# Attention, routed experts and a gated layer on one core: tokens stay in expert order for the gated stage, y turned by VectorE

## What is computed

```
kv  = einsum('bhsd,bhse->bhde', k, v)           # per batch and head, 64x64
o   = q @ kv;  x = o / sqrt(mean(o*o) + 1e-6) * g_norm       # N x 512
logits = x @ w_gate + modality_bias[modality_id]             # 8 experts
e = argmax(logits);  gate_w = softmax(logits)[e]
y[t] = gate_w[t] * (relu(x[t] @ w1[e]) @ w2[e])              # w1 512x1024
out = (sigmoid(y @ wg_gate) * (y @ wg_val)) @ w_out          # 512x1536, 1536x512
```

## Time and profile before

| | |
|---|---|
| three runs | 1637.22 to 1642.83 us, median 1638.06 |
| the profiled execution: span, first to last instruction | 1628.0 us; the runs' time also holds what lies before and after it, 10.1 us by the median |
| TensorE busy (its weight loads) | 1547.1 us, 95% (1297.4 us, 80%), 7924 instructions |
| VectorE, ScalarE, GpSimd busy | 559.8 us (34%), 397.9 us (24%), 181.3 us (11%) |
| first and second gated product (lines 1047, 1058) in the chain that ended last | 36% and 18% |

### The profile page before, as it was taken

How to read it: one execution, slowest core, us unless ns; L and a number is a source line. 1 busy time by engine, 2 the same in 40 slices (tenths; PEclk the granted TensorE clock), 3 DMA queues, 4 the chain that set the end, 5 groups by cost and what they waited for, 6 DMA issues and landing times.

```text
span 1628.0 us, 23019 instructions
## 1 busy us (share of the span) xinstructions
PE 1547.1 (95%) x7924; PEld 1297.4 (80%) x7925; DVE 559.8 (34%) x938; ACT 397.9 (24%) x744; POOL 181.3 (11%) x298
## 2 busy tenths in 40 slices
PE   6988479999999999969999999999999999999998
PEld 5878368888888888858888888888888888888886
DVE  2877743364524552233312212122121221212111
ACT  2766112222222222233221211112111121111111
POOL 1443122222222222100000000000000000000000
PEclk9999589999999999989999999999999999999999
DMA  9998223243314332043110000101001010010000
GB/s 226 257 266 232 81 75 106 71 154 129 120 47 136 112 128 64 31 134 103 65 52 1 30 23 1 53 1 52 1 1 52 1 52 1 0 52 0 27 0 26
DMA packets 56321, 120.61 MB, mean 74 GB/s; under 512 B 7614, under 2 KB 32190, under 8 KB 55488
## 3 DMA queue, kind: packets, MB, share of 16 engines
q1 hardware_dynamic: 49856, 99.75, 20.9%
q0 software_dynamic: 6400, 19.93, 4.0%
HBM read 91.33 MB, written 29.38 MB: 74 GB/s over the span
## 4 chain that ended last, share of the span: by engine, by line
PE 58%; issue 25%; DMA 6%; POOL 4%; POOLq 3%; DVE 1%; SPq 1%; ACT 0%; DVEq 0%; ACTq 0%
PE ps L1047 36%; PE ps L1058 18%; DMA vt<-in_v 4%; POOL xg L477 3%; POOLq L476 2%; PE ps L942 1%; PE ps L911 1%; PE ps L1037 1%; DMA raw<-in_moe_w 1%; POOL hold L471 1%; POOL from_now L475 1%; POOLq L484 0%; DMA x_rows<-xb 0%; DVE ssum L714 0%; POOL y_rows L485 0%
## 5 line engine op out<-in xcount | busy, mean ns | idle before, releaser
L1047 PE MATMUL ps<-yhi,gv 128*128 128x512 f32 x1728 | 548.1, 389 | 1.5 <-DVE ylo L874 1.5
L1047 PEld LDWEIGHTS ps<-yhi,gv 128*128 128x128 f32 x1728 | 324.3, 188 | 69.2 <-issue 1.9
L1047 PE MATMUL ps<-ylo,gv 128*128 128x512 f32 x864 | 336.1, 389 | 0.0
L1058 PE MATMUL ps<-wo,shi 128*128 128x512 f32 x864 | 266.9, 390 | 1.4 <-DVE slo L892 1.4
L890 DVE TENSOR_TENSOR s<-ps,sig 128x512 f32<-128x512 f32 x108 | 74.7, 692 | 489.2 <-ACT sig L609 489.2
L992 PE MATMUL ps<-ew,xhi 128*128 x640 | 203.3, 399 | 2.2 <-DVE xlo L811 1.7
L1014 PE MATMUL ps<-ew,hhi 128*128 x640 | 197.2, 389 | 1.3 <-DVE hlo L822 1.3
L1058 PEld LDWEIGHTS ps<-wo,shi 128*128 128x128 f32 x864 | 161.5, 188 | 35.0 <-DVE slo L892 1.9
L1047 PEld LDWEIGHTS ps<-ylo,gv 128*128 128x128 f32 x864 | 162.2, 188 | 33.7
L609 ACT ACTIVATE sig<-ps 128x512 f32<-128x512 f32 x108 | 64.7, 599 | 500.5 <-PE ps L1047 500.5
L1058 PE MATMUL ps<-wo,slo 128*128 128x512 f32 x432 | 168.2, 389 | 0.0
(11 more groups left out here) (139 smaller groups left out, 1280.0 us busy)
## 6 DMA issues: line engine op xcount, KB each, us to landing
raw<-in_moe_w SPq DMA_DIRECT2D x64, 512.0 KB, 4.0
qt<-in_q SPq DMA_DIRECT2D x8, 1152.0 KB, 13.3
x_rows<-xb SPq DMA_DIRECT2D x8, 1152.0 KB, 15.0
yin<-y_rows SPq DMA_DIRECT2D x18, 512.0 KB, 5.5
out<-ot SPq DMA_DIRECT2D x18, 512.0 KB, 2.9
kt<-in_k SPq DMA_DIRECT2D x7, 1152.0 KB, 20.2
vt<-in_v SPq DMA_DIRECT2D x7, 1152.0 KB, 25.1
graw<-in_moe_w_gate SPq DMA_DIRECT2D x6, 512.0 KB, 3.6
```

What stands on the lines that cost most here:

```text
L1047: last = mm(ps[:, 2 * (f % 2) + part, :], gv[f // 2][:, w, part, d, cols], x[c % 2][:, d, :], start=first, stop=end)
L1058: last = mm(ps[:, 4 + m, :], s[:, rows], wo[f // 2][:, w, f % 2], start=(f == 0 and s is shi and w == 0), stop=(f == GC - 1 and s is slo))
```

## The change

- The 4608 rows of `y_rows` now lie in **expert order with the padding closed up**: row = place in the padded list minus the padding of the experts before. `compact_rows` works out `to_i` (five VectorE operations after xlo of tile 0). The scatter stores beside each row of y its token number in `row_tok`, by a second indirect DMA.
- **The gate** is applied to the expert tile, when y is copied out of PSUM. For that GpSimd gathers the 128 gates of a tile (`gather_gate`), and the gather of x two tiles on waits for it, since it overwrites `from_now`. The copy also writes the row in the order (g, c, i), 4 groups of 4x32 features.
- **y is turned by VectorE** in squares of 32x32 (`y_turned`): a block is loaded with 32 tokens by 4 groups on the partitions (four DMAs, runs of 512 B), and four transposes give `yt` in SBUF. TensorE's transposes and their special order go.
- **Block 0** is loaded, turned and split within the expert stage, after step 35 (`ahead_of`; ScalarE issues the loads). The first weight piece is loaded once all tiles but the last expert's are done, the second right after the first is split. `high` and `low` of a piece stand after the column instead of before it.
- **Output rows** are scattered to their tokens by four indirect DMAs per block, with `out_tok` loaded from `row_tok` (128x36 elements of 4 bytes).

```diff
@@ SP
-            sp.dma_start(gate_n[:], gates.rearrange("(b p m) -> p b m", p=128, m=4)).then_inc(gates_in, 16)
...
             def load_y(b):
-                for half in range(2):
-                    wait(sp, pe_yt, 4 * (b - 1) + 2 * half + 2)
-                    sp.dma_start(yin[:, half], y_v[bass.ds(b, 1), :, 2 * half:2 * half + 2, :].rearrange("a p m d -> p (a m) d")).then_inc(yin_in[half], 16)
+                sp.wait_ge(yt_made, 4 * b)
+                for g in range(4):
+                    sp.dma_start(yin[32 * g:32 * g + 32], y_v[b, g]).then_inc(yin_in, 16)
...
-            sp.wait_ge(pe_hT, tiles_used * 2)
+            tiles_early = sp.value_load(used[0:1, 1:2], min_val=E - 1, max_val=NT)
+            sp.wait_ge(pe_y, tiles_early)
             load_glu(0)
+            load_glu(1)
             sp.wait_ge(pe_y, tiles_used)
             for p in range(2):
-                sp.wait_ge(y_out[p], (tiles_used + (1 - p)) // 2 * 16)
-            load_y(0)
-            for n in range(1, PIECES):
+                sp.wait_ge(y_out[p], (tiles_used + (1 - p)) // 2 * 32)
+            load_glu(2)
+            sp.dma_start(out_tok[:], row_tok_v, allow_slow_non_contiguous=True).then_inc(tok_in, 16)
+            load_y(1)
+            for n in range(3, PIECES):
                 load_glu(n)
...
@@ GpSimd
             def gather(t):
+                wait(pool, gate_in[t.p], 16 * t.half)
                 when(pe_x, t.n - 1)
...
             def scatter(t):
                 when(y_made, t.n + 1)
                 nc.gpsimd.tensor_copy(to_now[:, t.p:t.p + 1], to_i[:, bass.ds(t.n, 1)])
+                nc.gpsimd.tensor_copy(tok_now[:, t.p:t.p + 1], from_i[:, bass.ds(t.n, 1)])
                 pool.drain()
                 nc.gpsimd.indirect_dma_start(
                     out=y_rows, out_offset=bass.IndirectOffsetOnAxis(ap=to_now[:, t.p:t.p + 1], axis=0),
                     in_=y[:, t.p], in_offset=None, bounds_check=N - 1, oob_is_err=False).then_inc(y_out[t.p], 16)
+                nc.gpsimd.indirect_dma_start(
+                    out=row_tok, out_offset=bass.IndirectOffsetOnAxis(ap=to_now[:, t.p:t.p + 1], axis=0),
+                    in_=tok_now[:, t.p:t.p + 1], in_offset=None, bounds_check=N - 1, oob_is_err=False).then_inc(y_out[t.p], 16)
+
+            def gather_gate(t):
+                nc.gpsimd.indirect_dma_start(
+                    out=gate_now[:, t.p:t.p + 1], out_offset=None, in_=gates,
+                    in_offset=bass.IndirectOffsetOnAxis(ap=from_now[:, t.p:t.p + 1], axis=0)).then_inc(gate_in[t.p], 16)
...
                     use(Tile(i, c - 1), scatter)
+                    use(Tile(i, c + 1), gather_gate)
...
+            pool.wait_ge(tok_in, 16)
+            for b in range(NB):
+                for m in range(4):
+                    pool.wait_ge(o_kept, 4 * b + m + 1)
+                    nc.gpsimd.indirect_dma_start(
+                        out=out, out_offset=bass.IndirectOffsetOnAxis(ap=out_tok[:, 4 * b + m:4 * b + m + 1], axis=0),
+                        in_=ot[:, m], in_offset=None).then_inc(o_out[m], 16)
@@ ScalarE
+            def load_first():
+                for p in range(2):
+                    act.wait_ge(y_out[p], 32 * ((BLK // 128 + E) // 2))
+                for g in range(4):
+                    act.dma_start(yin[32 * g:32 * g + 32], y_v[0, g]).then_inc(yin_in, 16)
+                y_high(0, 0)
@@ VectorE
             def y_of(t):
-                wait(dve, y_out[t.p], 16 * t.half)
+                wait(dve, y_out[t.p], 32 * t.half)
                 dve.wait_ge(pe_y, t.n + 1)
-                nc.vector.tensor_copy(y[:, t.p], ps[:, 5, :]).then_inc(y_made, 1)
+                dve.wait_ge(gate_in[t.p], 16 * (t.half + 1))
+                nc.vector.tensor_scalar(y[:, t.p].rearrange("p (g c i) -> p c g i", g=4, c=DC),
+                                        ps[:, 5, :].rearrange("p (c g i) -> p c g i", g=4, c=DC),
+                                        gate_now[:, t.p:t.p + 1], None, ALU.mult).then_inc(y_made, 1)
...
+            def y_turned(i, c):
+                b = 2 * i + c
+                dve.wait_ge(yin_in, 64 * (b + 1))
+                for m in range(4):
+                    nc.vector.transpose(yt[c % 2][:, :, 128 * m:128 * m + 128].rearrange("p c (t j) -> p t c j", j=32),
+                                        yin[:, 4 * m:4 * m + 4, :].rearrange("p t (c i) -> p t c i", i=32)).then_inc(yt_made, 1)
...
-                    if f == 8 and not last:
-                        y_gated(i, c + 1)
+                    if f == 9 and not last:
+                        dve.wait_ge(glo_made, 3 * PIECES)
+                        y_turned(i, c + 1)
```

More of the change, by code:

```diff
@@ L210, in moe_program @@
     assert glu.at <= ew_base + UNITS * 2 * 4096
-    yhi0 = glu("yhi0", [128, DC, BLK], F32R)
-    ylo0 = glu("ylo0", [128, DC, BLK], F32R)
-    yhi, ylo = [yhi0, yhi1], [ylo0, ylo1]
+    ahead = Place(SBUF_END - 3 * DC * BLK * 4)
+    assert ahead.at >= expert_place.at
+    yt1 = Place(glu.at - DC * BLK * 4)("yt1", [128, DC, BLK], F32)
+    yt0 = Place(ahead.at)("yt0", [128, DC, BLK], F32)
+    ylo0 = ahead("ylo0", [128, DC, BLK], F32R)
+    yhi0 = ahead("yhi0", [128, DC, BLK], F32R)
+    yin = ahead("yin", [128, BLK // 32, 128], F32)
+    yhi, ylo, yt = [yhi0, yhi1], [ylo0, ylo1], [yt0, yt1]
     low_part = Place(glu_base)
@@ L227, in moe_program @@
     slo = small("slo", [128, BLK], F32R)
-    yin = small("yin", [128, 2, 2, D])
-    ot = small("ot", [128, 2, 2, D])
+    ot = small("ot", [128, 4, D])
+    assert glu.at <= SBUF_END - 3 * DC * BLK * 4
     ctx = ExitStack()
@@ L332, in __call__, with tiles @@
                         stage(t, *args)
-        def tiles(engine, step):
+        def tiles(engine, step, ahead_of=None):
             step(0, 0, False)
@@ L339, in tiles @@
                     step(i, c, True)
-            for n in range(FULL - 1, NT + 1):
+            step(0, FULL - 1, True)
+            if ahead_of:
+                ahead_of()
+            for n in range(FULL, NT + 1):
                 step(0, n, True)
@@ L601, in block_step @@
                 for f in range(GC):
-                    if first and f % 2 == 0 and f // 2 + 1 < PIECES:
-                        high(f // 2 + 1)
                     if f == 10 and not last:
@@ L612, in block_step @@
                     nc.scalar.copy(shi[:], s32[:]).then_inc(shi_made, 1)
+                    if first and f % 2 == 0 and f // 2 + 1 < PIECES:
+                        high(f // 2 + 1)
                     if f == 0 and not first:
@@ L781, in _ @@
                 one_hot(r_low, r_lo, 128, n, 1).then_inc(hot_made, 1)
+            then(nc.vector.scalar_tensor_tensor(out=r_spare[:], in0=r_nt[:], scalar=128.0, in1=ps[:, 1, 0:E], op0=ALU.mult, op1=ALU.subtract))
             dve.wait_ge(pe_table, 1)
@@ L892, in block_step @@
                     nc.vector.tensor_tensor(slo[:], s32[:], shi[:].bitcast(F32), ALU.subtract).then_inc(slo_made, 1)
+                    if first and f % 2 == 0 and f // 2 + 1 < PIECES:
+                        low(f // 2 + 1)
             low(0)
-            dve.wait_ge(gates_in, 16)
-            y_gated(0, 0)
-            y_low(0, 0)
             blocks(dve, block_step)
@@ L1029, in _ @@
             tiles(pe, tile_step)
-            def y_transposed(i, c, half):
-                b = 2 * i + c
-                pe.wait_ge(yg_made, 4 * b + 2 * half + 2)
-                for m in range(2 * half, 2 * half + 2):
-                    for d in range(DC):
-                        last = nc.tensor.transpose(ps[:, m, 128 * d:128 * d + 128], yin[:, half, m % 2, 128 * d:128 * d + 128], ident[:])
-                    last.then_inc(pe_yt, 1)
             def gate_value(i, c, f):
```

144 lines of the change are left out of this document (69 added, 75 removed).

## The result

The changed kernel takes **1836.19 us** (median of 4 runs, 1829.23 to 1837.71), the kernel before 1637.64 us (4 runs, 1635.13 to 1642.83: the three of the first section and one beside the changed kernel): a ratio of **1.121**, 95% interval 1.118 to 1.125. That is 12% slower, where 1622.7 was predicted, and outside the range.

The account below looks back on a forecast made before the run. TensorE was taken as the bound, busy for 487.2 of 489 us in the expert stage. Terms -14.3 - 12.0 + 1 + 3.5 + 5 + 1.4 from 1628.0 gave 1612.6, carried over to 1622.7 us; range 1610 to 1648.

Parts of the forecast that it names:

- Scatter, two small indirect DMAs, gather: Expert stage, GpSimd: the added small DMAs issue x later, delaying some tiles with weight loads; +5 us, bounds 0 and 22.
- d: Expert stage: excess of x's arrival over 12.07 us after the hold, delaying every second step by d; forecast 0.33 us.
- The text's own signs of being wrong: Row_tok 3 us behind y, expert steps over 13 us, TensorE waiting in block 0, or expert stage growing over 25 us.
- The clock: Seam to the gated stage: a clock drop during the new standstill slows some matmuls; +1 us, bounds 0 and 3.
- Transposes: Gated stage: TensorE's 16 transposes of y go in 8 block changes, VectorE's replacements cost nothing; -14.3 us.
- The seam: Between expert and gated stages: block 0 and weights ready early, shortening TensorE's standstill; -12.0 us, bounds -10 and -12.5.
- Block 0 loaded early: Tile 36 of the expert stage: work queues behind block 0's loads and transposes, delaying ReLU; +3.5 us, bounds 0 and 6.
- Tail: End of the kernel: four indirect stores replace two plain ones; +1.4 us, bounds 0.5 and 8.
- Carried over: Whole kernel: the 10.1 us by which the median of three runs exceeded the profiled span, added to the forecast.
- Rival 1: Expert stage: indirect DMAs each wait for the previous landing, tiles take 15.2 to 17.8 us; 1734 to 1830 us, chance 0.12.
- Rival 2: Expert stage: gates land as slowly as large gathers (5.3 us), TensorE waits every second step; 1630 to 1668 us, chance 0.20.
- Rival 3: Block 0 of the gated stage: late weight pieces or slow transposes take back the seam's gain; 1627 to 1640 us, chance 0.08.

Follow-up runs that it names:

- e1_no_tok: The changed kernel with the scatter of token numbers to row_tok left out, output rows staying in expert order: 1638.09 us.
- e3: The changed kernel with both the scatter to row_tok and the gather of gates, with its waits, left out: 1630.88 us.
- f1_tok_in_row: The changed kernel with the token number carried as an extra word in the row of y, one scatter, no row_tok: 1639.59 us.
- e5_wide: The changed kernel with each token number written 16 times, 64 bytes a row, to row_tok: 1663.04 us.
- b0_before: The kernel before, unchanged, profiled once more on the same chip as its companions: 1631.37 us.
- f3: f1_tok_in_row with gates gathered by their own index behind the gather of x, which no longer waits for them; block 0 as in the change: 1629.28 us.
- e2_no_gate: The changed kernel without the gather of gates and both waits for it (all gates 1), row_tok kept: 1752.17 us.
- g5_before_side: The kernel before plus, behind each scatter of y, an unread scatter of 4-byte constants to words side by side: 1793.12 us.
- g2: The kernel before plus, behind each scatter of y, an unread scatter of 4-byte constants spread by token number: 1657.06 us.

## Why the prediction was wrong, point by point

- **The step that failed** is "Scatter, two small indirect DMAs, gather": +5 us, bounds 0 and 22; measured +216. It reads "A small gather isn't in the trace: between 2.1 us ... and 5.9 ...; I take 2.4". For gates by themselves that was right: 2.7 in e1_no_tok, and all small DMAs but row_tok cost 6 us of the stage (e1 less e3). The fault is that row_tok got an issue of 1.05 us and no landing at all. Both things behind it wait for that landing: gates, which come in with it or after it, and the drain ahead of x and of y, whose wait the text had itself read off ("Something waits for the landing: the drain ahead of each, or the DMA itself"). With a landing of 8.7 us in place of nothing, gates are in at +11.7 by the medians (issued at +4.2, 7.5 us); with the text's 1.5 us to the issue of x and a median landing of 3.5, x comes at +16.7 instead of +12.4, and d is 4.6 instead of 0.33. In the long pair above x comes at +22.5 and d is 10.5. By the text's formula, over 37 tiles, that is 86 us and 194 us; TensorE's waits for xg after the first tile are 143 us, between the two, and the slower clock adds its 60. The text's own signs of being wrong came true: turns of x stand 13.3 to 23.6 us apart from 242.35 on, and the stage grows by more than 25. Even the text's own far bound of 5.9 us for a small landing, put on row_tok (issued at +2.45), would have let the drain go at +9.2, x land at +12.5 to +15.1, and cost 37 x 0.4 / 2 to 37 x 3.0 / 2, 7 to 55 us: the sign would have been open.
- **The clock** was looked at in the seam only (+1, measured +3: the first 48 matmuls 14.08 us against 11.13 in the chain of before). In the expert stage its fall to 0.88 adds some 60 us to the waits. No term had it.
- **Transposes, -14.3**: they are gone, and the gated stage is 8.5 shorter. The first matmuls take back 3; the 0.03 us by which each of 108 columns is longer takes 3.2. Why a column is longer was not tested; over long stretches of f1_tok_in_row and e5_wide it was 8.26 to 8.40.
- **The seam, -12.0**: -11.0 against the profiled execution, -9.5 against b0_before, whose seam is 15.8. The missing 1 us of the new seam is the branches between y and the first subtraction.
- **Block 0 loaded early, +3.5, bounds 0 and 6**: the wait for h is 5.6 to 6.7 wherever the stage runs nearly on time (f1, e3, e1, f3). The loads land in 9.9 us (median of e3), above the 8.7 that was taken as their worst. In the change itself the wait is 0.3 us, as TensorE is late anyway.
- **Tail, +1.4, bounds 0.5 and 8**: +3.7. The first issue is 0.3 us later than forecast, the four are 1.28 us apart instead of 1.02 (0.8 more), and from the last issue to the end of the span are 4.5 us instead of the 3.2 of the text (2.8 + 0.4): 2.4 more in all.
- **Carried over, +10.1**: what lies around the span is 1.8, as b0_before shows; the other 8.3 only set the forecast against the median instead of the quick profiled execution, and no error comes of it.
- **Rival 1** (DMAs in line), 1734 to 1830 us: nearly the right time and the wrong mechanism. Its sign was that row_tok leaves 3 us behind y; it leaves 1.33 behind. Its other half, that something waits for each landing, was true of the drain. **Rival 2** (the gate's round trip ends last) is what GpSimd's waits show (273.5 us for gates), but e2_no_gate shows that the drain would have waited without it; and its price was that of a slow gather, while gates alone land in 2.7. **Rival 3**: TensorE waits for neither weights nor ylo in block 0; the read of 4608 words landed in 8.3 us, hidden. The lock between VectorE and GpSimd is there (hold 0.71 us at 258.55 against 0.20 at 242.69) and small.

## What to carry to other kernels

Give every DMA that a change adds two prices, its issue and its landing, and ask of each drain and wait behind it whether it now waits for that landing; a DMA whose data nobody reads still holds up the next one (g5_before_side). Small per-row data that is written by index goes into the row that is written anyway, or at a pitch, not into words side by side; here the row is the better place (stage 509.6 against 534.6). A step that a buffer frees just in time (here 1.9 us of slack in 12.24) turns each late landing into a wait, and waits spread over a stage can cost more than their sum, since TensorE's clock may fall with them (here 156 us of waits, 60 us of slower work).

## What the runs showed of the hardware that was not expected

- 128 indexed writes of 4 bytes land in 8.7 to 8.8 us when they lie side by side, and in the steps shown hold the drain up for only 1.69 us in place of 7.72 when they are spread (g2 against g5); writing 64 bytes in place of each 4 made the scatter faster, not slower.
- DMAs issued beside such a scatter land late, on other queues too: gates 7.5 us instead of 2.7 (after, e1), SP's weight loads 8.7 instead of 3.4 (g5, before), and gates 11.2 to 13.6 where both meet.
- GpSimd issues indirect DMAs 1.28 to 1.49 us apart when no drain stands between (after, expert stage and end); with a drain the next one waits for the landing, plus 0.8 us.
- ScalarE's four loads of y (256 KB each, 512-byte pieces) land in 10.0 us (median, after), beside the first gated weights; the same loads from SP, one block later each, in 5.2.
